# Attention in front of two feed-forward layers: sixteen units of a head pair over a whole batch become thirty-two over half a batch

## The reference, cut to what matters

```
q_d, k_d, v_d = means over groups of 4 tokens
out_up = repeat(softmax(q_d @ k_d.T / 8) @ v_d, 4)
scores = where(|i - j| < 4, q @ k.T / 8, -1e9)
x = out_up + softmax(scores) @ v          # as (2304 tokens, 512)
h = relu(x @ w_in)                        # 512 -> 2048
x = (s * h * h + b) @ w_out               # 2048 -> 512
out = ((x @ w_a) * (x @ w_b)) @ w2        # 512 -> 1536 -> 512
```

## Time and profile before

| | |
|---|---|
| median of 3 runs (1069.66 to 1070.23) | 1070.12 us |
| profiled execution: its own time, and its span | 1069.81 us, 1068.0 us |
| PE busy | 1009.2 us, 94% |
| DVE, ACT, POOL busy | 442.6, 356.3, 159.4 us |
| mean granted TensorE clock, share of full speed | 0.974 |
| chain that ended last: PE, DVE, ACT, POOL | 85, 6, 3, 3% |

### The profile page before, as it was taken

How to read it: one execution, slowest core, us unless ns; L and a number is a source line. 1 busy time by engine, 2 the same in 40 slices (tenths; PEclk the granted TensorE clock), 3 DMA queues, 4 the chain that set the end, 5 groups by cost and what they waited for, 6 DMA issues and landing times.

```text
span 1068.0 us, 17004 instructions
## 1 busy us (share of the span) xinstructions
PE 1009.2 (94%) x6984; PEld 944.7 (88%) x6984; DVE 442.6 (41%) x800; ACT 356.3 (33%) x791; POOL 159.4 (15%) x126
## 2 busy tenths in 40 slices
PE   5678899999999999999999799999999999999997
PEld 4557889999999999999999699899899898998996
DVE  4768665565555655554345521211211212112111
ACT  3445444444344443344245421211211212212211
POOL 4545343122331223310000000000000000000000
PEclk9659999999999999999999899999999999999999
DMA  7343401121011210201033600010100100100000
GB/s 193 77 124 112 126 20 50 45 68 46 17 52 46 68 46 15 55 13 43 10 111 119 200 1 1 20 40 1 57 3 1 60 1 1 60 1 1 30 2 30
DMA packets 98829, 52.50 MB, mean 49 GB/s; under 512 B 60384, under 2 KB 92768, under 8 KB 98752
## 3 DMA queue, kind: packets, MB, share of 16 engines
q1 hardware_dynamic: 98608, 51.35, 17.3%
q10 hardware_dynamic: 144, 0.07, 0.0%
HBM read 41.97 MB, written 9.44 MB: 48 GB/s over the span
## 4 chain that ended last, share of the span: by engine, by line
PE 85%; DVE 6%; ACT 3%; POOL 3%; issue 2%; DMA 1%; SPq 0%; ACTq 0%; DVEq 0%; POOLq 0%
PE bank L667 28%; PE bank L632 18%; PE bank L617 17%; PE bank L681 13%; PE bank L546 2%; PE bank L493 2%; PE bank L517 2%; PE bank L467 1%; DVE relu L992 1%; POOL sm L1073 1%; PE bank L478 1%; POOL sm L1081 1%; PE bank L538 1%; POOL wx L1088 1%; PE bank L512 1%
## 5 line engine op out<-in xcount | busy, mean ns | idle before, releaser
L667 PE MATMUL bank<-x_hi,wx 128*128 128x384 f32 x1152 | 307.0, 337 | 11.8 <-DVE prod L1051 7.8
L632 PE MATMUL bank<-g_hi,wx 128*128 128x288 f32 x1024 | 234.2, 305 | 1.4 <-DVE o_sb L1004 1.4
L617 PE MATMUL bank<-wx 128*128 128x288 f32 x1536 | 230.7, 299 | 0.4 <-ACT relu L792 0.4
L667 PEld LDWEIGHTS bank<-x_hi,wx 128*128 128x128 f32 x1152 | 210.2, 188 | 17.3 <-issue 14.4
L617 PEld LDWEIGHTS bank<-wx 128*128 128x128 f32 x1536 | 211.8, 190 | 3.4 <-issue 2.8
L667 PE MATMUL bank<-x_lo,wx 128*128 128x384 f32 x576 | 193.5, 336 | 0.0
L632 PEld LDWEIGHTS bank<-g_hi,wx 128*128 128x128 f32 x1024 | 171.9, 189 | 9.5 <-issue 4.2
L1051 DVE TENSOR_TENSOR prod<-bank,a_sb 128x384 f32<-128x384 f32 x72 | 40.1, 558 | 314.5 <-ACT a_sb L854 314.5
L632 PE MATMUL bank<-g_lo,wx 128*128 128x288 f32 x512 | 151.5, 296 | 0.0
L992 DVE SCALAR_TENSOR_TENSOR relu<-relu,s_col 128x288 f32<-128x288 f32 x128 | 81.7, 638 | 166.4 <-ACT relu L792 166.2
L854 ACT ACTIVATE a_sb<-bank 128x384 f32<-128x384 f32 x72 | 35.3, 491 | 303.7 <-PE bank L667 303.7
(11 more groups left out here) (67 smaller groups left out, 821.4 us busy)
## 6 DMA issues: line engine op xcount, KB each, us to landing
nat<-in_q SPq DMA_DIRECT2D x32, 144.0 KB, 2.9
nat<-in_k SPq DMA_DIRECT2D x32, 144.0 KB, 3.2
vnat<-in_v SPq DMA_DIRECT2D x32, 144.0 KB
o_transposed<-o_sb SPq DMA_DIRECT2D x8, 576.0 KB, 3.2
o_raw<-o_transposed SPq DMA_DIRECT2D x6, 768.0 KB, 4.7
out<-y SPq DMA_DIRECT2D x18, 256.0 KB, 2.2
vwin<-in_v SPq DMA_DIRECT2D x32, 120.0 KB
raw<-in_moe_w_a SPq DMA_DIRECT2D x12, 256.0 KB, 3.1
```

Source lines behind the costliest of these rows:

```text
L617: mm = nc.tensor.matmul(HB[:, 0:HALF], wi(w, kd, f), xs(x, c % 2)[:, kd], start=(kd == 0 and j == 0), stop=(kd == KD - 1 and j == 2))
L632: mm = nc.tensor.matmul(ACC[o][:, 0:HALF], wo(w, f, o), g[:, slot % GB, :], start=(f == 0 and j == 0), stop=(f == F1 - 1 and j == 2))
L667: mm = nc.tensor.matmul(dst[:, 0:CH2], wab(w, f, j * KD + kd), x[:, kd, :], start=(kd == 0 and m == 0), stop=(kd == KD - 1 and m == 2))
```

## The change

The unit `u` is now a head pair over half a batch: 32 units, four for each chunk. A unit makes pooled scores for its 72 pooled queries and local scores for its three windows. Keys and pooled values belong to the pair: the unit of a batch's first half (`leads(u)`) turns and pools the keys, and the later unit finds them in `kT` and `pooledk`. Only the four units of the first half of batch 0 run ahead of slot 0, and four weight blocks instead of six are split there. Each of the other 28 is laid over four slots, at ticks 0 to 11 counted from `start(u)`, a new one every 8 ticks. POOL's subtraction is gone: DVE negates the maxima, and ACT takes six exponentials of 102 columns with the negated maximum as bias and the sum from the accumulator. ACT instead of DVE copies the pooled result (`take_up`). In the second layer, six weight blocks are split beside the first layer's last slots, and the others one at a time behind the first steps' own work; before, blocks 6 to 8 were split between the layers.

```diff
-BOOT_BLOCK_TICKS = (10, 14, 18, 22, 25, 28)
+PER_UNIT = 2 * F1 // PAIRS
+LEAD = 5
+BOOT_SKEW = 4
+BOOT_TICKS = 23
+BOOT_BLOCK_TICKS = (-16, -12, -8, -4)
...
+EARLY2 = 6
...
+        def start(u):
+            return BOOT_SKEW * u - BOOT_TICKS if alone(u) else PER_UNIT * (u - PAIRS) - LEAD
+
+        def at_tick(g, t):
+
+            return [u for u in range(NU) if start(u) + t == g]
...
+            def attention(g):
+                for u in at_tick(g, 9):
+                    values(u)
+                for u in at_tick(g, 7):
+                    turn_local(u)
+                for u in at_tick(g, 5):
+                    turn_pooled(u)
+                for u in at_tick(g, 3):
+                    scores(u)
+                for u in at_tick(g, 0):
+                    if leads(u):
+                        turn_k(u)
+                for u in at_tick(g, 1):
+                    turn_q(u)
...
+            def exp_local(u):
+                act.wait_ge(shiftl_ready, u + 1)
+                for j in range(2 * GW):
+                    x = kits[kit(u)]["sml"][:, j, 0:WK]
+                    done = nc.scalar.activation(x, x, ACT.Exp, bias=shiftl(u)[:, j:j + 1], accum_out=denl(u)[:, j:j + 1])
+                done.then_inc(el_ready, 1)
...
+                for u in at_tick(g, 10):
+                    take_up(u)
+                for u in at_tick(g, 8):
+                    take_local(u)
+                for u in at_tick(g, 6):
+                    take_pooled(u)
+                for u in at_tick(g, 0):
+                    if leads(u):
+                        take_k(u)
+                for u in at_tick(g, 1):
+                    take_q(u)
+                for u in at_tick(g, 4):
+                    exp_pooled(u)
+                for u in at_tick(g, 5):
+                    exp_local(u)
...
-            for f in range(6, 9):
-                split_w2_hi(f)
...
+                    if c == 0 and EARLY2 + f < F2:
+                        split_w2_hi(EARLY2 + f)
...
+                nc.vector.tensor_tensor(x, src, rows, ALU.add).then_inc(masked, 1)
+                dve.wait_ge(masked, u + 1)
+                nc.vector.tensor_reduce(mxl(u), kits[kit(u)]["sml"][:, :, 0:WK], X, ALU.max).then_inc(mxl_ready, 1)
+                dve.wait_ge(mxl_ready, u + 1)
+                nc.vector.tensor_scalar(shiftl(u), mxl(u), -1.0, None, ALU.mult).then_inc(shiftl_ready, 1)
+                dve.wait_ge(sp_ready, u + 1)
+                src = bank[0:GH, at + 2, 0:2 * G].rearrange("p (e c) -> p e c", e=2)
+                nc.vector.tensor_reduce(mxp(u), src, X, ALU.max).then_inc(mxp_ready, 1)
+                dve.wait_ge(mxp_ready, u + 1)
+                nc.vector.tensor_scalar(shift(u), mxp(u), -1.0 / POOL ** 2, None, ALU.mult).then_inc(shift_ready, 1)
...
-            def subtract(n, kind):
...
+            for slot in range(SLOTS):
+                c, f = divmod(slot, F1)
+                attention(2 * slot)
+                attention(2 * slot + 1)
+                if c == 0 and f + BOOT_BLOCKS < F1 and f % 2 == 1:
+                    split_w_lo(f + BOOT_BLOCKS)
```

More of the change, by code:

```diff
@@ L220, in past @@
                 eng.wait_ge(semaphore, count)
[L223 to L237, removed]
-            return JOBS * n + kind + 1 if n >= 0 else 0
-        def local(n, kind):
-            return 2 * n + kind if n >= 0 else 0
-        def nat(n):
-            return (nat0, nat1)[kit(n)]
@@ L306, in pt_bank, with place, leads, pair @@
-        def pt_bank(n):
-            return 4 * kit(n) + 2 if alone(n) else 1
-        def o_bank(n, kind):
-            return 4 * kit(n) + (1 if kind == LOCAL0 else 0) if alone(n) else 0
-        def boot_tick(at, tick_of):
-            return [p for p in range(PAIRS) if at - BOOT_SKEW * p == tick_of]
+        def place(u):
+            return u // (2 * PAIRS), u // PAIRS % 2, u % PAIRS
+        def leads(u):
+            return place(u)[1] == 0
+        def pair(u):
+            i, _, p = place(u)
+            return PAIRS * i + p
@@ L457, in _ @@
         def _(pe):
-            def turn(n, t):
-                if t == 0:
-                    pe.wait_ge(nat_in[kit(n)], 64 * uses(n))
-                    past(pe, o_taken, job(before(n), LOCAL1))
-                    past(pe, pt_taken, job(before(n), LOCAL1))
-                if t == 3 and not alone(n):
-                    pe.wait_ge(turn_taken, 4 * n + 1)
-                for u in range(GW):
-                    mm = nc.tensor.transpose(bank[:, turn_bank(n, t), u * WQ:(u + 1) * WQ],
-                                             nat(n)[:, t // 2, GW * (t % 2) + u, :], ident[0:WQ, 0:WQ])
-                mm.then_inc(turn_ready, 1)
@@ new lines, in attention @@
+            def attention(g):
+                for u in at_tick(g, 11):
+                    split_x_lo(u)
+                for u in at_tick(g, 10):
+                    take_values(u)
+                for u in at_tick(g, 6):
+                    weigh_local(u)
+                for u in at_tick(g, 4):
+                    weigh_pooled(u)
+                for u in at_tick(g, 1):
+                    if leads(u):
+                        sum_k(u)
+                for u in at_tick(g, 2):
+                    sum_q(u)
+                for u in at_tick(g, 3):
+                    maxima(u)
@@ L1036, in _ @@
                         split_w2_lo(f // 2 - 2)
-            for f in range(6, 9):
-                split_w2_lo(f)
             take_acc(NCH - 1)
@@ L1124 @@
+            for g in range(-BOOT_TICKS, 0):
+                attention(g)
+                if g in BOOT_BLOCK_TICKS and BOOT_BLOCK_TICKS.index(g) % 2 == 1:
+                    split_w_lo(BOOT_BLOCK_TICKS.index(g))
+            for slot in range(SLOTS):
+                c, f = divmod(slot, F1)
+                attention(2 * slot)
+                attention(2 * slot + 1)
+                if c == 0 and f + BOOT_BLOCKS < F1 and f % 2 == 1:
+                    split_w_lo(f + BOOT_BLOCKS)
 _INS = ['q', 'k', 'v', 'moe_w_in', 'moe_w_out', 'moe_s', 'moe_b', 'moe2_w_a', 'moe2_w_b', 'moe2_w_out']
```

947 lines of the change are left out of this document (386 added, 561 removed).

## The result

The changed kernel takes 1160.39 us (median of 4 runs, 1158.4 to 1161.52), the kernel before 1070.17 (4 runs, 1069.66 to 1071.5). The ratio is 1.0839, with a 95% interval of 1.082 to 1.0858: slower, by about 90 us. The forecast was 1165. The profiled execution took 1160.05 us, and its span is 1157.3.

The account below looks back on a forecast made before the run. PE, busy 94% of the span, was taken as the bound. Start-up 70, slots 408.3, units 177.8, keys 15.6, chunk 0 25, accumulators 2 and second layer 463.7 gave 1162.4; plus 1.8, stated as 1165, range 1132 to 1200 (8 in 10: 1105 to 1203).

Parts of the forecast that it names:

- S to P: From a unit's scores to its pooled-weight turn: chain 4.6 us against 3.35 of PE cover, so PE waits 1.2.
- P to L: From the pooled turn's slot to the local-weight turn: chain 2.95 us against cover 1.6, so PE waits 1.3.
- Q to S: From the query turn's slot to the scores: chain 2.1 us against cover 1.6, so PE waits 0.45.
- Keys: Key turn of leading units waits for ACT's copy of the local weights: 1.3 us for 12 of 28 units.
- Own work of a unit: PE's work for one half-size unit under slots, without waits: 3.4 us.
- Chunk 0: Late pooled weights behind POOL's weight block 16 us, slower clock 5, missing cover in slots 0 and 1 4; together 25.
- Start-up: Before slot 0: rounds of 13.4 us, first up matmuls at 70 instead of 74.1 us, bounds 62 and 78.
- Seam: Between the layers: 6.56 us wait shrinks to about 1.1, plus 2.8 from the clock; gain 8.2 us.
- Half of the waits: Rival: 1.5 us less for each unit and 8 less in chunk 0, so 1115 us; chance 0.17.
- All hidden: Rival: every chain fits its cover, units cost 3.92 us, total 1070.6, or 1062 with start-up at 62; chance 0.12.
- The clock rival: Rival: each unit's waits pull PE's clock down, 2.8 us for each of 28 units, so 1243 us; chance 0.08.
- this rule: Skill's account of waits between short matmul groups repeatedly halving PE's clock; forecast charged nothing for it outside chunk 0.

Follow-up runs that it names:

- second run: Changed kernel with only the turn of the local weights moved behind the next slot's up matmuls; 1119.76 us.
- fourth run: Changed kernel with DVE taking pooled maxima and their negation ahead of the mask and local maxima; 1151.08 us.
- first run: Changed kernel with only the turn of the pooled weights moved from ahead of its slot's up matmuls to behind them; 1137.36 us.
- third run: Changed kernel with the key turn and ACT's copy of it moved to the head of a later slot, ahead of the values; 1144.57 us.
- eleventh run: Changed kernel with pooled, local and key turns later, POOL's weight block later, pooled query sum earlier, pooled maxima first, start-up local exponentials earlier; 1047.48 us, 0.9795 of kernel before.
- ninth run: Changed kernel with only POOL's chunk 0 weight block moved behind the next pooled weights instead of ahead; 1149.47 us.
- eighth kernel: Changed kernel with pooled, local and key turns moved later and POOL's chunk 0 weight block behind the pooled weights; 1066.9 us.
- seventh run: Kernel before with only the second layer's weight blocks 6 to 11 split one at a time behind the first steps; 1062.79 us, ratio 0.9933.
- fifth run: Changed kernel with the old arithmetic back: POOL subtracts the maxima, ACT takes one exponential of 612 columns, DVE sums; 1225.47 us.
- sixth run: Kernel before with only the six exponentials with bias and accumulated sum, no subtraction, no DVE sum; 1078.34 us, ratio 1.0083.

## Why the prediction was right, point by point

The forecast, with its own mechanism, held: 1165 against 1160.39. Its sum closes term by term against the span of 1157.3 (the forecast's was 1162.4). That it came within 0.4% is in part luck: the errors of the single terms, all counted as positive, come to some 27 us (9 for the units, 6 for the keys, 4 for chunk 0, the rest smaller), and all but 5 of that cancelled. The mechanism is not luck: the waits stand where the forecast put them, each within 0.1 us of its price.

| term | forecast | measured | from |
|---|---|---|---|
| first up matmuls | 70 | 71.4 | windows |
| a unit | 6.35 | 6.03 | 18.79 - 12.76 |
| a key turn on top | 1.3 | 1.82 | 20.61 - 18.79 |
| chunk 0 above steady | 25 | 20.7 | 97.7 - 3 x 18.79 - 20.61 |
| last 16 slots | 51 + 2 | 55.0 | windows |
| second layer | 463.7 | 465.2 | 1157.3 - 692.1 |

*S to P* (1.2): the idle time is 1.02 (24.7 us over the 24 turns of chunks 1 to 6), and with the 0.17 of the second run a wait costs 1.19. Chain and cover were nearly as added up from the rows: from the last pooled score (421.21) to the turn (425.89) it is 4.68 us, forecast 4.6, and PE's own work in between is 3.49, forecast 3.35. The fourth run shows that the chain ends last (0.27 less of it, 0.25 less of the group), the first that the wait goes when the turn gets one more set of up matmuls as cover.

*P to L* (1.3): 1.05 idle, 1.25 by the second run. From the start of the down matmuls (409.04) the chain is 2.80 us and the cover 1.58, forecast 2.95 and 1.6. That `weigh_local` stands behind P's square, and that the exponentials cost nothing, is in the timeline. The first run shows how near the edge that is: with PE 1 us earlier the exponentials hold the relu.

*Q to S* (0.45): 0.22 idle, about 0.4 as a cost, the least of the terms. (The forecast's own numbers add up to 2.17 - 1.6 = 0.57.)

*Keys* (1.3): exactly what the third run took away. But I had put the turn's own work into a mean for all units, and it is 0.5 more for those that follow a key turn. With 12 of them this is 6 us too little.

*Own work of a unit* (3.4): the eleventh run has no waits left in its middle and groups of 16.0: 3.25. So 3.25 + 1.19 + 1.25 + 0.39 = 6.08, against 6.03 measured and 6.35 forecast; each term came out a little under its forecast, 28 times, which is 9 us too much.

*Chunk 0* (25): the block in POOL's queue is right in kind (5.52 us at one turn, 17.7 in four), its price by the ninth run is 10.4, with the clock, where I had 16 and 5. The other 10.3 were to be 4, for slots 0 and 1; the eighth kernel, too, needs 78.2 where its steady groups would take 66.4. The granted clock was 0.88 over the 97.7 us of chunk 0, and the up matmuls of slots 0, 1, 4, 8 and 12 ran wholly or mostly at half of the full one (2.6 to 2.8 us from the first to the last start, 1.5 elsewhere). If PE alone held this chunk, that would be up to 97.7 x 0.12 = 11.7 us, an estimate. No run takes waits and clock apart there.

*Start-up* (70): the masks of the four units start at 11.51, 24.42, 37.96 and 51.35, so rounds take 12.9, 13.5 and 13.4 us. The forecast said 13.4, though the terms that it lists add up to 13.7.

*Seam* (8.2): 471.9 to 465.2 is 6.7 here, and 6.5 in the seventh run. The wait of 6.56 is now 1.26, in

```profile
697.72 0.41 PE L625 MATMUL bank<-x_hi,wx 128*128 128x384 f32 x1 [1.26 <-DVE prod L953]
```

That is 5.3, so only 1.4 came from the clock and its neighbours, not 2.8, though the clock is 1.00 in 692 to 716, as assumed.

*What the sum left out:* the two last sets of down matmuls behind slot 127, 3.2 us, which the earlier trace rows has in its 490 to 596 stretch. On the other side the units lead their slots by 5 ticks, so that the group of slots 108 to 111 holds no whole unit (15.70 instead of 18.79); that is 3.1. The two cancel. The last 16 slots, which hold those 3.2, took 2 us above their term.

*The range.* By its own terms (8 us of start-up, 0.75 and 0.85 us a unit) the forecast's range is 1136 to 1197, a little narrower than the 1132 to 1200 that it states.

*The rivals.* Half of the waits would have been 1.45 us a unit; they cost 2.8. All hidden is what the eighth kernel is, with another order. The clock rival is false for this kernel (1.00 in chunks 1 to 6, with two waits of 1.0 us in each unit). In part it is true for the fifth, where the clock fell behind 11 of 24 waits of 2.05 us, and for the first, where it fell three times. The Trainium skill ("TensorE: Matmul & The Clock Gate", "HAM oscillation — how this bites in real kernels") tells of a kernel whose clock fell again and again, at waits of some 3 to 5 us between short bursts of matmuls. The fifth run shows repeated falls with no wait above 2.06 us in chunks 1 to 6. The forecast said that by this rule the rival would hold; the waits that it expected were well under those of that kernel, so the rule did not bear on them. The forecast gave this rival 0.08. The old arithmetic in the new order, with waits 0.55 and 1.0 us longer, was enough to make it true in part.

*The word "exponential".* The prediction put the cost of the exponentials at nothing where they stood. That was right here, but it was not a property of theirs: they cost 9 us in the kernel before (the sixth run), where 2.2 us of them stand in front of a copy that PE waits for, and in place of the subtraction and the sum they gain 65 us in the new order, where both chains are short of time. With the turns moved as in the eighth run their worth was not measured. What stays open is which waits, in length and in closeness, made the clock fall in the fifth run, where it cost some 20 us; runs that change the length of one wait alone were not made.

## What to carry to other kernels

Halving a unit halves the work but not the chain, and halves the cover: set each chain, operation by operation, against what the bounding engine has to do between the chain's two ends. Where the chain is longer, every unit waits for the difference. Before giving up a finer tiling, move the waiting operations one set of matmuls later; here that was worth 93 us. A replacement on a mostly idle engine has a price by what stands behind it in that engine's queue, and the same replacement cost 0.8% in one kernel and gained over 5% in the other.

## What was not expected of the hardware

- A wait of the list costs some 0.17 us more than its idle time, as the second run works out.
- In the fifth run the clock fell to half behind 11 waits of 2.05 us, each in the first unit after a key turn, and stayed at 1.00 behind 13 others as long. In the changed kernel waits of 1.0 to 1.1 us, twice per 18.8, left it at 1.00.
- DVE's negation of 72x2 elements took 0.91 us instead of 0.17 beside a GpSimd subtraction; the low part (L909) took 774 ns in the mean instead of 552, and up to 1.30 beside `sml` on POOL (1.15 in the mean for the 52 that overlap an operation of POOL, 0.51 for the other 76), while the square (L905) went from 638 to 523 ns, since only 2 of 128 now overlap POOL's work and 22 did before.
- Six exponentials of 102 columns, each 0.37 us long, start 0.36 us apart, with the reads of their sums (0.19 each) in between. Each read starts 0.27 us behind its exponential, and the next exponential 0.09 behind the read. What the six would take without the reads no run shows.
